# Windowed attention on one core: own keys and window keys in separate 128-column blocks

## Chip, cores and metric

One Trainium2 chip, one of its cores. The metric is the device time of one execution in microseconds; the median of the runs stands for a kernel. Profiled times count from the start of the span that the profiler records.

## What is computed

Two batches of 768 rows pass through an attention, a gated convolution block and a second one. Only the attention is touched by the change.

```
scores = scale * q @ k.T                       # 8 heads of 64
is_global = pos[None, :] < n_global            # 8
is_local  = (rel >= 0) & (rel < n_local)       # 96
dist = where(is_global & ~is_local, n_local, abs(rel))
scores = where(keep, scores - slopes * dist, -1e9)
a = softmax(scores)
x = a @ v                                      # attention
gate = sigmoid(causal conv(x)); y = (gate * (x @ w_val)) @ w_out
h = relu(y @ w_in); out = (h * sigmoid(conv(h))) @ w_out2
```

Query row r sees the 8 global keys and the last 96 rows up to itself.

## The kernel before

The 2 x 768 rows are 12 tiles of 128 queries, 6 a batch. For a tile the keys are 232: the previous tile's last 96 (PREV), the tile's own 128, and the 8 global ones (GLOB). For the first tile of a batch (tiles 0 and 6) they are 128. All matrix products are fp32, or split into a high and a low part.

The layout cuts the 232 keys of a tile in another place than the tiles do. kW holds previous 96, own 128, global 8 in this order. OLD = 104 of them are "old": the previous 96 and the tile's own first 8. The other NEW = 128 are the tile's own keys 8 to 127 and the global 8. Old keys are seen only by the tile's first 104 queries. So `turn` transposes the old part of each head as 104 x 104, and `pv` adds its product to 104 query columns only. v is stored to match: v_new (own rows 8 to 127, then the global 8) takes two loads, v_old (previous 96, own 8) two more. probT holds both parts of two heads side by side in 464 columns.

Each engine has its program written out by hand. One round t of the loop is, on TensorE, `qk(t + 1)` (scores of the next tile, 8 heads), `turn(t, j)` for four pairs of heads, `pv(t)`. VectorE takes the scores out of PSUM with bias and minimum (L951), copies turned pairs 1 and 3 (`copy_t1`, L958), takes x out (L974), and makes the inverse of the sums (total_eps L962, reciprocal, a small transpose). ScalarE does the exponentials (L701) and copies pairs 0 and 2 (L708). Three PSUM banks serve four pairs, so pair 3 waits for the copy of pair 0. GpSimd copies the window's keys from tile to tile (`key_window`, L384, L385), splits w2 (L397, L399), splits x for the next stage (L405, L407) and multiplies x by the inverse (`scale_x`, L391). SyncE issues all loads in one order; in a round it sends the inverse to memory, loads v, q and k of later tiles and loads the inverse back, spread out.

Ahead of the loop stands a product of two weights, w1t by win, on TensorE (L469, L454), fed by part loads on SyncE's and ScalarE's queues. SyncE waits for the third part of both (`w1_in[2]`) before it loads wval and the second half of win. VectorE makes the tables of biases in that time (L1057 to L1074), then low parts of weights (L931, L926). Behind the loop TensorE does dense products to the end.

Of the kernel before, what the change touches and what calls it, by code (L numbers as in the profile page):

```python
# [6 lines left out]
P = 128  # L7
C = H * D
# [11 lines left out]
KEYS = PREV + P + GLOB  # L20
OLD = PREV + GLOB
NEW = KEYS - OLD
BAND = PREV + P
# [20 lines left out]
def program(nc, A_q, A_k, A_v, A_n, A_wval, A_w1t, A_win, A_w2, A_cw1, A_cw2, A_out):  # L44
# [7 lines left out]
    with ctx:  # L52
# [62 lines left out]
        v_new = sb("v_new", [P, RING, C], where=am)  # L115
        v_old = sb("v_old", [P, RING, C], where=am)
# [5 lines left out]
        probT = sb("probT", [P, PAIRS, 512], where=am)  # L122
# [7 lines left out]
        rel, loc = probT[:, 0, 0:KEYS + GLOB], probT[:, 0, KEYS + GLOB:2 * (KEYS + GLOB)]  # L130
        notloc, lt = probT[:, 1, 0:KEYS + GLOB], probT[:, 1, KEYS + GLOB:2 * (KEYS + GLOB)]
        dist, dist_first = probT[:, 2, 0:KEYS], probT[:, 2, KEYS:KEYS + P]
        key, glob, dglob = (probT[:, 3, i * GLOB:(i + 1) * GLOB] for i in range(3))
# [134 lines left out]

        @block.sync
        def _(sp):  # L270
# [4 lines left out]
            sp.wait_ge(w1_in[2], 32)  # L275
# [958 lines left out]
```

## Time and profile before

| | us |
|---|---|
| median of 3 runs | 265.56 |
| lowest and highest | 265.42, 266.8 |
| the profiled execution's own time | 265.42 |
| its span | 263.6 |

| engine | busy us | share of the span |
|---|---|---|
| TensorE, matmul | 256.9 | 97% |
| TensorE, weight load | 203.7 | 77% |
| VectorE | 187.5 | 71% |
| ScalarE | 149.1 | 57% |
| GpSimd | 46.5 | 18% |

TensorE's granted clock is full over the whole span. An fp32 product shows as two records of weight load and two of matmul, a turn (transpose) as one of each. A matmul's duration holds its way through the array too, so for what one costs the others the starts are read, not the durations. Durations of GpSimd are rough.

### The profile page before, as it was taken

What the parts mean: (1) busy time and instruction counts of PE and PEld (TensorE: products, weight loads), DVE (VectorE), ACT (ScalarE), POOL (GpSimd) and SP (SyncE); (2) the same over time, 40 slices, a digit from 0 to 9 for tenths busy, and PEclk for the clock granted to TensorE, in tenths of its full rate; (3) what the DMA queues carried; (4) which work ended last, traced back from release to release, by engine and by line L of the source; (5) the groups of instructions that cost most, each with busy time, mean ns of one, the idle gap of its engine ahead of it and who ended that gap; (6) DMA issues with size and microseconds to landing.
All of it is one profiled execution on the core that took longest, in us unless ns stands there. A gap on an engine that the chain in (4) does not pass through costs nothing.

```text
span 263.6 us, 4429 instructions
## 1 busy us (share of the span) xinstructions
PE 256.9 (97%) x1526; PEld 203.7 (77%) x1526; DVE 187.5 (71%) x468; ACT 149.1 (57%) x346; POOL 46.5 (18%) x71
## 2 busy tenths in 40 slices
PE   8999999999999899999999999999999999999995
PEld 7544468889678788888888888888888888888883
DVE  0388389998999969989833979987319989991000
ACT  1061578999989755263634328965447559752100
POOL 1002157793568512000000000000000000000000
PEclk9999999999999999999999999999999999999999
DMA  6799957779785111000000000000000004004021
GB/s 203 258 357 275 308 169 223 222 211 258 224 260 149 46 55 31 2 1 2 0 0 0 0 2 0 1 0 2 0 0 0 2 0 159 0 0 162 0 107 53
DMA packets 24635, 24.67 MB, mean 94 GB/s; under 512 B 3732, under 2 KB 16532, under 8 KB 24484
## 3 DMA queue, kind: packets, MB, share of 16 engines
q1 hardware_dynamic: 23460, 23.37, 29.2%
q10 hardware_dynamic: 1152, 1.01, 1.1%
q8 instruction: 13, 0.21, 0.3%
q14 instruction: 10, 0.08, 0.1%
HBM read 21.03 MB, written 3.34 MB: 92 GB/s over the span
## 4 chain that ended last, share of the span: by engine, by line
PE 88%; DVE 8%; issue 2%; ACT 1%; ACTq 0%
PE ps L561 21%; PE ps L563 21%; PE ps L562 21%; PE ps L454 9%; PE ps L501 4%; DVE prob L951 4%; PE ps L528 4%; PE ps L515 2%; PE ps L532 2%; PE ps L516 2%; PE ps L469 1%; PE ps L465 1%; DVE total_eps L962 1%; DVE probT L958 1%; DVE xT L974 1%
## 5 line engine op out<-in xcount | busy, mean ns | idle before, releaser
L701 ACT ACTIVATE prob<-prob,low 128x232 f32<-128x232 f32 (+1 forms) x96 | 44.3, 466 | 6.9 <-DVE low L951 6.7
L979 DVE SCALAR_TENSOR_TENSOR g<-xT,cw,g 128x512 f32<-128x512 f32 x48 | 34.9, 793 | 1.6 <-ACT g L736 1.6
L807 ACT ACTIVATE h<-ps 128x512 f32<-128x512 f32 x24 | 14.0, 596 | 31.2 <-PE ps L563 31.1
L951 DVE CUSTOM_DVE_ANT_0 prob<-ps,bias 128x232 f32<-128x232 f32 x80 | 28.4, 383 | 1.4 <-PE ps L501 1.3
L561 PE MATMUL ps<-gh,Wh 128*128 128x512 f32 x64 | 24.9, 389 | 0.0
L562 PE MATMUL ps<-gl,Wh 128*128 128x512 f32 x64 | 24.9, 389 | 0.0
L563 PE MATMUL ps<-gh,Wl 128*128 128x512 f32 x64 | 24.9, 389 | 0.0
L561 PE MATMUL ps<-hghA,w2h 128*128 128x512 f32 x64 | 24.9, 389 | 0.0
L562 PE MATMUL ps<-hglA,w2h 128*128 128x512 f32 x64 | 24.9, 389 | 0.0
L563 PE MATMUL ps<-hghA,w2l 128*128 128x512 f32 x64 | 24.9, 389 | 0.0
L454 PE MATMUL ps<-win,w1t 128*128 128x512 f32 x56 | 24.5, 594 | 0.0
L1141 DVE SCALAR_TENSOR_TENSOR hgA<-h,cw,hgA 128x512 f32<-128x512 f32 x32 | 21.8, 745 | 3.6 <-ACT hgA L819 3.6
L501 PE MATMUL ps<-kW,q_rows 64*128 64x232 f32 (+1 forms) x192 | 20.7, 355 | 0.0
L516 PE MATMUL ps<-ident,prob 128*128 128x128 f32 x96 | 20.3, 275 | 0.4 <-ACT probT L708 0.3
L454 PEld LDWEIGHTS ps<-win,w1t 128*128 128x128 f32 x56 | 10.6, 190 | 12.6 <-issue 12.4
L528 PE MATMUL ps<-probT,v_new 128*64 128x128 f32 x192 | 19.3, 282 | 1.0 <-DVE probT L958 0.9
L561 PE MATMUL ps<-xh,wvh 128*128 128x512 f32 x48 | 19.0, 395 | 0.3 <-issue 0.3
L501 PEld LDWEIGHTS ps<-kW,q_rows 64*128 64x128 f32 x192 | 16.6, 186 | 3.0 <-issue 1.1
L562 PE MATMUL ps<-xl,wvh 128*128 128x512 f32 x48 | 18.7, 390 | 0.0
L563 PE MATMUL ps<-xh,wvl 128*128 128x512 f32 x48 | 18.7, 390 | 0.0
L515 PE MATMUL ps<-ident,prob 104*104 104x104 f32 x80 | 17.8, 260 | 0.9 <-ACT probT L708 0.9
L701 ACT ACTIVATION_READ_ACCUMULATOR prob<-prob,low 128x1 f32 x96 | 18.3, 191 | 0.0
(105 smaller groups left out, 545.6 us busy)
## 6 DMA issues: line engine op xcount, KB each, us to landing
q_rows<-in_q SPq DMA_DIRECT2D x12, 256.0 KB, 4.3
kW<-in_k SPq DMA_DIRECT2D x12, 256.0 KB, 5.0
v_new<-in_v SPq DMA_DIRECT2D x12, 240.0 KB
invT<-inv_turned SPq DMA_DIRECT2D x20, 128.0 KB, 3.3
out<-xT SPq DMA_DIRECT2D x5, 512.0 KB, 2.8
w<-in_w SPq DMA_DIRECT2D x8, 256.0 KB, 9.7
v_old<-in_v SPq DMA_DIRECT2D x10, 192.0 KB
prob<-in_wval SPq DMA_DIRECT2D x1, 1024.0 KB, 4.8
```

The costliest lines, as they stand in the source:

```text
L454: return pe.matmul(WB(i), w1t[:, m, k * P:(k + 1) * P], win[:, m, half * 512:(half + 1) * 512], start=(m == 0), stop=(m == CT - 1))
L501: last = pe.matmul(SC(f, i % 2)[:, i // 2, OLD if first_of_batch(t) else 0:KEYS], q_rows[rows, slot, pair, :], keys, start=True, stop=True)
L515: pe.transpose(PT(t, j)[0:OLD, at:at + OLD], head[0:OLD, 0:OLD], ident[0:OLD, 0:OLD])
L516: last = pe.transpose(PT(t, j)[:, at + OLD:at + KEYS], head[:, OLD:KEYS], ident[:, :])
L528: last = pe.matmul(PO[rows, j, :], v_new[:, slot, cols], probT[:, j, e * KEYS + OLD:(e + 1) * KEYS], start=True, stop=first_of_batch(t))
L561: pe.matmul(out, w_hi, x_hi, start=first, stop=False)
L562: pe.matmul(out, w_hi, x_lo, start=False, stop=False)
L563: return pe.matmul(out, w_lo, x_hi, start=False, stop=final)
L701: act.activation(part, part, ACT.Exp, scale=-1.0, bias=low[:, t % 2, i:i + 1], accum_out=total[:, t % 2, i:i + 1]).then_inc(exp_done, 1)
L951: dve.tensor_tensor_reduce(prob[:, t % 2, i, cols], SC(f, e)[:, i % HH // 2, cols], table, -SCALE, 3.0e38, ALU.add, ALU.min, low[:, t % 2, ...
L979: dve.scalar_tensor_tensor(out=pieces(g[:, m, :], c), in0=x_cols(m, c, tap - PAD1), scalar=cw1[:, m, tap:tap + 1], in1=pieces(g[:, m, :], ...
L1141: dve.scalar_tensor_tensor(out=raw, in0=h_cols(m, c, tap - 1), scalar=cw2[:, m, tap:tap + 1], in1=raw, op0=ALU.mult, op1=ALU.add).then_inc ...
```

## The change

The keys of a tile are cut where the tiles are cut. The window (WIN = 104) is now the global 8 and the previous 96, the rest are the tile's own 128 keys in their order. kW holds window and own part in that order. v is held as v_own (128 rows, one load) and v_win (96 and 8 rows, two loads); the first tile of a batch has v_own only. The turned parts lie in blocks of 128 columns: `turn` transposes the 104 window keys for all 128 queries, and `pv` multiplies window and own part for all 128 queries, the window first. The copies out of PSUM take 512 columns where they took 464. The tables of biases are built over other slices, with one operation and one iota fewer. SyncE's wait for `w1_in[2]` ahead of wval is gone.

```diff
 GLOB, PREV = 8, 96
-KEYS = PREV + P + GLOB
-OLD = PREV + GLOB
-NEW = KEYS - OLD
-BAND = PREV + P
+WIN = GLOB + PREV
+KEYS = WIN + P
...
-        probT = sb("probT", [P, PAIRS, 512], where=am)
+        probT = sb("probT", [P, HALVES, HH, 2, P], where=am)
...
         def turned(t, j):
-            both = PT(t, j)[:, 0:2 * KEYS]
-            return both.rearrange("p (i k) -> p i k", i=2)[:, :, OLD:KEYS] if first_of_batch(t) else both
+            rows = PT(t, j).rearrange("p (i c q) -> p i c q", i=2, c=2)
+            return rows[:, :, 1, :] if first_of_batch(t) else rows.rearrange("p i c q -> p (i c q)")
...
-            sp.wait_ge(w1_in[2], 32)
             sp.dma_start(wval, A_wval).then_inc(wv_in, 16)
...
-                sp.dma_start(v_new[0:P - GLOB, slot, :], A_v[GLOB:P, t, :]).then_inc(v_in[slot], 16)
-                sp.dma_start(v_new[P - GLOB:P, slot, :], A_v[0:GLOB, t // TPB * TPB, :]).then_inc(v_in[slot], 16)
+                sp.dma_start(v_own[:, slot, :], A_v[:, t, :]).then_inc(v_in[slot], 16)
                 if not first_of_batch(t):
-                    sp.dma_start(v_old[0:PREV, slot, :], A_v[P - PREV:P, t - 1, :]).then_inc(v_in[slot], 16)
-                    sp.dma_start(v_old[PREV:OLD, slot, :], A_v[0:GLOB, t, :]).then_inc(v_in[slot], 16)
+                    sp.dma_start(v_win[GLOB:WIN, slot, :], A_v[P - PREV:P, t - 1, :]).then_inc(v_in[slot], 16)
+                    sp.dma_start(v_win[0:GLOB, slot, :], A_v[0:GLOB, t // TPB * TPB, :]).then_inc(v_in[slot], 16)
...
                 for i in range(2):
-                    head, at = prob[:, t % 2, 2 * j + i, :], i * KEYS
-                    if not first_of_batch(t):
-                        pe.transpose(PT(t, j)[0:OLD, at:at + OLD], head[0:OLD, 0:OLD], ident[0:OLD, 0:OLD])
-                    last = pe.transpose(PT(t, j)[:, at + OLD:at + KEYS], head[:, OLD:KEYS], ident[:, :])
+                    for c in key_parts(t):
+                        keys = slice(WIN, KEYS) if c else slice(0, WIN)
+                        last = pe.transpose(PT(t, j)[0:keys.stop - keys.start, (2 * i + c) * P:(2 * i + c + 1) * P],
+                                            prob[:, t % 2, 2 * j + i, keys], ident[:, :])
...
-                    heads = [(e, slice((2 * j + e) * D, (2 * j + e + 1) * D), slice(e * D, (e + 1) * D)) for e in range(2)]
-                    for e, cols, rows in heads:
-                        last = pe.matmul(PO[rows, j, :], v_new[:, slot, cols], probT[:, j, e * KEYS + OLD:(e + 1) * KEYS],
-                                         start=True, stop=first_of_batch(t))
-                    if not first_of_batch(t):
-                        for e, cols, rows in heads:
-                            last = pe.matmul(PO[rows, j, 0:OLD], v_old[0:OLD, slot, cols], probT[0:OLD, j, e * KEYS:e * KEYS + OLD],
-                                             start=False, stop=True)
+                    for c in key_parts(t):
+                        v, keys = (v_win, v_own)[c], (WIN, P)[c]
+                        for e in range(2):
+                            cols = slice((2 * j + e) * D, (2 * j + e + 1) * D)
+                            last = pe.matmul(PO[e * D:(e + 1) * D, j, :], v[0:keys, slot, cols], probT[0:keys, j // 2, j % 2 * 2 + e, c, :],
+                                             start=(c == key_parts(t)[0]), stop=(c == 1))
...
-                link(dve.scalar_tensor_tensor(out=dist[:, 0:BAND], in0=notloc[:, 0:BAND], scalar=MASKED,
-                                              in1=loc[:, 0:BAND], op0=ALU.mult, op1=ALU.add))
-                link(dve.tensor_copy(dist[:, BAND:KEYS], dglob))
-                link(dve.tensor_copy(dist_first[:, 0:BAND - OLD], dist[:, OLD:BAND]))
-                link(dve.tensor_tensor(dist_first[:, BAND - OLD:NEW], notloc[:, KEYS:KEYS + GLOB], dglob, ALU.mult))
-                link(dve.tensor_tensor(dist_first[:, BAND - OLD:NEW], dist_first[:, BAND - OLD:NEW], loc[:, KEYS:KEYS + GLOB], ALU.add))
+                link(dve.tensor_tensor(dist_first, notloc[:, own], dglob, ALU.mult))
+                link(dve.tensor_tensor(dist_first, dist_first, loc[:, own], ALU.add))
+                link(dve.tensor_copy(dist[:, 0:GLOB], dglob[:, 0:GLOB]))
+                link(dve.scalar_tensor_tensor(out=dist[:, window_keys], in0=notloc[:, window_keys], scalar=MASKED,
+                                              in1=loc[:, window_keys], op0=ALU.mult, op1=ALU.add))
```

TensorE, tile 1, the last turns and the first two pairs of `pv`, before. A row names the line, the output and the inputs, and the output's rows by columns; "x2" is two heads.

```order
L515 MATMUL ps<-ident,prob 104x104
L516 MATMUL ps<-ident,prob 128x128
L528 MATMUL ps<-probT,v_new 64x128 x2
L532 MATMUL ps<-probT,v_old 64x104 x2
L528 MATMUL ps<-probT,v_new 64x128 x2
```

The same place in the changed kernel:

```order
L517 MATMUL ps<-ident,prob 104x128
L517 MATMUL ps<-ident,prob 128x128
L532 MATMUL ps<-probT,v_win 64x128 x2
L532 MATMUL ps<-probT,v_own 64x128 x2
L532 MATMUL ps<-probT,v_win 64x128 x2
```

The count is the same; the window part comes first in `pv`, and its rows go from 104 to 128 columns.

SyncE, one round's loads with the inverse's way out and back (L303, L311), before:

```order
L303 DMA inv_turned<-inv_rows 4x32x32
L294 DMA v_new<-in_v 120x512
L295 DMA v_new<-in_v 8x512
L297 DMA v_old<-in_v 96x512
L298 DMA v_old<-in_v 8x512
L283 DMA q_rows<-in_q 128x512
L288 DMA kW<-in_k 128x4x128
L311 DMA invT<-inv_turned 64x4x128 x2
```

The same round in the changed kernel:

```order
L307 DMA inv_turned<-inv_rows 4x32x32
L299 DMA v_own<-in_v 128x512
L301 DMA v_win<-in_v 96x512
L302 DMA v_win<-in_v 8x512
L288 DMA q_rows<-in_q 128x512
L293 DMA kW<-in_k 128x4x128
L315 DMA invT<-inv_turned 64x4x128 x2
```

One load stands fewer ahead of q, k and the inverse.

## Rows read from the trace of the kernel before

**Rows 1.** The page's chain that ended last: shares of the span by engine.

```profile
PE 88%; DVE 8%; issue 2%; ACT 1%; ACTq 0%
```

**Rows 2.** Busy time by stretch: length, then each engine (x instructions), clock, DMA share, GB/s.

```profile
43.89:49.27 5.38, 5.38 (x67) 4.68 (x66) 4.89 (x22) 4.88 (x19) 3.96 (x6) 1.00 0.82 235
...
64.75:70.13 5.38, 4.89 (x46) 3.56 (x48) 5.01 (x23) 4.98 (x20) 2.23 (x4) 1.00 0.82 231
70.13:75.45 5.32, 5.21 (x64) 4.26 (x60) 5.29 (x22) 5.10 (x18) 3.44 (x5) 1.00 0.82 239
...
107.00:250.00 143.00, 143.00 (x633) 118.44 (x632) 103.81 (x146) 76.77 (x106) 0.00 (x0) 1.00 0.04 15
```

**Rows 3.** Timeline of the weight loads in round 7: start, us, what, [idle before].

```profile
73.97 0.20 PEld L528 LDWEIGHTS ps<-probT,v_new 128*64 128x64 f32 x4 [0.31 <-DVE probT L958]
```

**Rows 4.** Timeline of TensorE in round 2, three turns in a row.

```profile
45.84 0.25 PE L515 MATMUL ps<-ident,prob 104*104 104x104 f32 x1
45.93 0.27 PE L516 MATMUL ps<-ident,prob 128*128 128x128 f32 x1
46.04 0.25 PE L515 MATMUL ps<-ident,prob 104*104 104x104 f32 x1
```

**Rows 5.** The chain at 92 us: start, us, what.

```profile
92.02 0.18 PE ps L532 x4
92.20 0.22 PE ps L528 x4
```

**Rows 6.** Groups by line and shape: the copies out of PSUM on VectorE.

```profile
L958 DVE COPY probT<-ps 128x464 f32<-128x464 f32 x20 | 12.8, 639 | 2.5 <-PE ps L516 2.4
...
L958 DVE COPY probT<-ps 128x256 f32<-128x256 f32 x4 | 1.7, 419 | 0.0
```

**Rows 7.** Timeline of VectorE in rounds 6 to 10: total_eps and one conv step.

```profile
66.42 0.85 DVE L962 TENSOR_SCALAR total_eps<-total 128x8 f32<-128x8 f32 x1
...
71.35 1.09 DVE L962 TENSOR_SCALAR total_eps<-total 128x8 f32<-128x8 f32 x1
...
77.13 0.17 DVE L962 TENSOR_SCALAR total_eps<-total 128x8 f32<-128x8 f32 x1
...
82.80 0.85 DVE L962 TENSOR_SCALAR total_eps<-total 128x8 f32<-128x8 f32 x1
...
86.86 1.69 DVE L979 SCALAR_TENSOR_TENSOR g<-xT,cw,g 128x512 f32<-128x512 f32 x1
```

**Rows 8.** Timeline of GpSimd in the same rounds.

```profile
65.97 1.28 POOL L391 TENSOR_TENSOR xT<-xT,invT 128x512 f32<-128x512 f32 x1 [0.56 <-DMA invT<-inv_turned]
...
71.13 1.28 POOL L407 TENSOR_TENSOR xl<-xT,xh 128x512 fp32r<-128x512 f32 x1
...
77.23 1.28 POOL L407 TENSOR_TENSOR xl<-xT,xh 128x512 fp32r<-128x512 f32 x1
...
86.73 1.27 POOL L391 TENSOR_TENSOR xT<-xT,invT 128x512 f32<-128x512 f32 x1
```

**Rows 9.** Timeline of SyncE's queue in round 6, one of four v loads.

```profile
69.07 0.31 SPq L295 DMA_DIRECT2D v_new<-in_v  x1
```

**Rows 10.** The start: timeline rows, one DMA issue, and one group by shape.

```profile
7.93 17.33 PE L454 MATMUL ps<-win,w1t 128*128 128x512 f32 x40
...
9.40 0.33 SPq L276 DMA_DIRECT2D prob<-in_wval  x1
...
21.78 3.07 DVE L926 TENSOR_TENSOR Wl<-ps,Wh 128x512 fp32r<-128x512 f32 x5
...
25.19 0.97 PEld L501 LDWEIGHTS ps<-kW,q_rows 64*128 64x128 f32 x16 [0.76 <-DVE Wl L926]
...
33.34 1.48 PEld L501 LDWEIGHTS ps<-kW,q_rows 64*128 64x128 f32 x16 [0.76 <-issue]
...
prob<-in_wval SPq DMA_DIRECT2D x1, 1024.0 KB, 4.8
...
L1057 DVE TENSOR_SCALAR probT<-probT,nval 128x240 f32<-128x240 f32 x1 | 0.3, 345 | 2.6 <-POOL probT L414 2.6
```

More of the change, by code:

```diff
@@ L114, in program @@
         q_rows = sb("q_rows", [P, RING, PAIRS, P], where=am)
-        v_new = sb("v_new", [P, RING, C], where=am)
-        v_old = sb("v_old", [P, RING, C], where=am)
+        v_own = sb("v_own", [P, RING, C], where=am)
+        v_win = sb("v_win", [P, RING, C], where=am)
         bias = sb("bias", [P, H, KEYS], where=am)
@@ L129, in program @@
         wval = prob[:, :, :, :].rearrange("p s i k -> p (s i k)")[:, 2 * H * KEYS - CT * C:2 * H * KEYS].rearrange("p (t c) -> p t c", t=CT)
[L130 to L133, printed above, removed]
+        rel = probT[:, 0, 0:2, :, :].rearrange("p a b c -> p (a b c)")[:, 0:KEYS]
+        loc = probT[:, 0, 0:2, :, :].rearrange("p a b c -> p (a b c)")[:, KEYS:2 * KEYS]
+        notloc = probT[:, 0, 2:4, :, :].rearrange("p a b c -> p (a b c)")[:, 0:KEYS]
+        key = probT[:, 0, 2:4, :, :].rearrange("p a b c -> p (a b c)")[:, KEYS:2 * KEYS][:, 0:P]
+        glob = probT[:, 1, 0:2, :, :].rearrange("p a b c -> p (a b c)")[:, 0:P]
+        dglob = probT[:, 1, 0:2, :, :].rearrange("p a b c -> p (a b c)")[:, P:2 * P]
+        lt = probT[:, 1, 0:2, :, :].rearrange("p a b c -> p (a b c)")[:, KEYS:2 * KEYS]
+        dist = probT[:, 1, 2:4, :, :].rearrange("p a b c -> p (a b c)")[:, 0:KEYS]
+        dist_first = probT[:, 1, 2:4, :, :].rearrange("p a b c -> p (a b c)")[:, KEYS:KEYS + P]
         attention_memory.close()
@@ L255, in first_of_batch, with key_parts @@
             return t % TPB == 0
+        def key_parts(t):
+            return (1,) if first_of_batch(t) else (0, 1)
         def v_landed(t):
-            return 16 * sum(2 if first_of_batch(u) else 4 for u in range(t % RING, t + 1, RING))
+            return 16 * sum(1 if first_of_batch(u) else 3 for u in range(t % RING, t + 1, RING))
         def turned(t, j):
-            both = PT(t, j)[:, 0:2 * KEYS]
-            return both.rearrange("p (i k) -> p i k", i=2)[:, :, OLD:KEYS] if first_of_batch(t) else both
+            rows = PT(t, j).rearrange("p (i c q) -> p i c q", i=2, c=2)
+            return rows[:, :, 1, :] if first_of_batch(t) else rows.rearrange("p i c q -> p (i c q)")
         def turned_to(t, j):
-            both = probT[:, j, 0:2 * KEYS]
-            return both.rearrange("p (i k) -> p i k", i=2)[:, :, OLD:KEYS] if first_of_batch(t) else both
+            part = probT[:, j // 2, j % 2 * 2:j % 2 * 2 + 2, :, :]
+            return part[:, :, 1, :] if first_of_batch(t) else part.rearrange("p i c q -> p (i c q)")
         @block.sync
@@ L499, in qk @@
                         pair, rows = 2 * f + i // 2, slice(i % 2 * D, i % 2 * D + D)
-                        keys = kW[rows, slot, pair, OLD if first_of_batch(t) else 0:KEYS]
-                        last = pe.matmul(SC(f, i % 2)[:, i // 2, OLD if first_of_batch(t) else 0:KEYS], q_rows[rows, slot, pair, :], keys,
+                        keys = kW[rows, slot, pair, P if first_of_batch(t) else P - WIN:2 * P]
+                        last = pe.matmul(SC(f, i % 2)[:, i // 2, WIN if first_of_batch(t) else 0:KEYS], q_rows[rows, slot, pair, :], keys,
                                          start=True, stop=True)
@@ L1055, in _ @@
             with dve.If(banded(dve)):
-                dve.wait_ge(iotas, 3)
+                dve.wait_ge(iotas, 2)
+                own, window_keys = slice(WIN, KEYS), slice(GLOB, KEYS)
                 link(dve.tensor_scalar(lt, rel, n_local, None, ALU.is_lt))
```

20 lines of the change are left out of this document (9 added, 11 removed).

## Prediction

> **What bounds the kernel now.** I read the chain of waits first, to see which engine carries the end [rows 1]. TensorE has 88% of it, VectorE 8%, so I asked next in which stretches VectorE stands in it. I call "round t" what TensorE does in one step of the attention loop: the scores of tile t+1, the turns (transposes) of tile t, its product with v. The busy time by stretch [rows 2] gives round 2 (43.89 to 49.27 us): TensorE 5.38 of 5.38 us, VectorE 4.89. Rounds 1 to 5 are like it. In rounds 6 (64.75) and 7 (70.13) TensorE has gaps, VectorE is busy 5.01 and 5.29 us and ScalarE 4.98 and 5.10: there the chain runs over VectorE. A wait of 0.31 us of TensorE for VectorE's copy in round 7 shows it [rows 3]. Behind the loop TensorE is busy 143.00 of 143.00 us [rows 2], so whatever the attention loop gains or loses by then reaches the end in full.
>
> **TensorE's columns.** For the ten tiles that have a window (all but 0 and 6) the key part of 104 is turned with 128 moving columns instead of 104, and the v part gets 128 query columns instead of 104. The timeline of round 2 shows three starts [rows 4]: the 104-column turn at 45.84, the 128-column one at 45.93, the next 104-column one at 46.04. So a turn of 104 columns holds the engine 0.09 us and one of 128 columns 0.11 us. Eight heads by 0.02 is 0.16 us a tile. In the chain [rows 5], four records of v_old (two heads side by side, 104 columns) take 0.18 us, four of v_new (128 columns) 0.22. Four pairs by 0.04 is 0.16 us. The last turn pair of a round waits about 0.1 us for ScalarE's copy of the first, since it reuses its PSUM bank; the added columns fill about 0.04 of that. A windowed tile costs TensorE 0.16 + 0.16 - 0.04 = 0.28 us. That the v_own product now follows v_win, and that accumulation starts with the window, changes no count and no weight; I cost it at nothing, with bounds of 0.02 us a pair either way, the size of the gaps that the rows can't resolve.
>
> Another reading of these gaps would be that weight loads set them: then the turns would stay as they are, and the sum would be 0.12 us less in each of rounds 1 to 5, 8 and 11, some 0.85 us. Against it: the short gap of 0.09 us is the one in which the 128 weight columns of the next turn are loaded, and the long one of 0.11 that in which 104 are. The Trainium skill, "TensorE: Matmul & The Clock Gate", section "LDWEIGHTS (loading the stationary operand)", has a load take its columns over 1.2 GHz, whatever the rows: an estimate of 107 ns for 128 columns and 87 for 104. By it the turns would cost nothing more. The trace has the long and the short gap the other way round, so I don't follow it here.
>
> **The copies out of PSUM.** They grow from 464 to 512 columns. VectorE takes 639 ns at 464 columns and 419 at 256 [rows 6]: 1.06 ns a column, so 48 more are 0.05 us each, two a tile. ScalarE's copies grow by the same columns, and I take the same 0.05, two a tile. For tiles 0 and 6 they stay at 2 x 128. In round 2 VectorE has 5.38 - 4.89 = 0.49 us of room, and the round gets 0.28 longer, so the copies hide.
>
> **The path, round by round.** Rounds 1 to 5 are TensorE's: 5 x 0.28 = 1.40. Round 0 and round 6 turn first tiles: nothing. In round 7 TensorE waits for VectorE's copies: two copies (0.10) and the last product (0.04), 0.14. Over rounds 8 to 10 the chain goes from TensorE to VectorE in round 9 and stays there until the last scores of tile 11 free the banks for the next stage: two copies in each of rounds 8 to 10, less what waited for TensorE anyway, 3 x 0.10 and up to 0.10 of turns ahead of a copy: 0.40. Tile 11 is turned between dense products, on TensorE alone: 0.28. Sum 1.40 + 0.14 + 0.40 + 0.28 = 2.22 us.
>
> **The port that VectorE and GpSimd share.** VectorE's total_eps works on 8 columns and should take some 0.17 us, as in round 8 (77.13). It took 0.85 in round 6 and 1.09 in round 7, and the conv step (usually 0.79) took 1.69 in round 10 [rows 7]. In rounds 6 and 7 it ends at 67.27 and 72.44, right where GpSimd's tensor_tensor ends (65.97 + 1.28 = 67.25; 71.13 + 1.28 = 72.41); in round 10 the conv step starts 0.13 us after GpSimd's multiply at 86.73 [rows 8]. These waits are 0.68 + 0.92 + 0.90 us, with one of 0.68 in round 9 (0.85 at 82.80) like them, and all four stand in the chain. What sets GpSimd's phase is in the diff: each of its operations there follows a k tile or an inverse that SyncE sends, after the v loads of the same step. One v load fewer takes 0.31 us off SyncE's queue [rows 9]. And two rounds of TensorE that are 0.28 longer lie between the moment GpSimd's inverse for round 6 is sent and VectorE's total_eps there. So GpSimd comes 0.31 + 0.56 = 0.87 us earlier against VectorE; its multiply started 0.45 us before total_eps and ran 0.83 into it, so the wait of round 6 should be gone. Not all of that reaches the end: the exponentials on ScalarE, busy 4.98 and 5.10 us in rounds 6 and 7, keep the next total_eps from following, and in round 7 it still meets a GpSimd operation. I take 0.64 us for both rounds (of 0.68 in round 6, with round 7's collision kept at what ScalarE leaves), between nothing and 1.6 (both waits).
>
> The Trainium skill has this as a rule, in "SBUF — State Buffer", section "Who interferes with whom": VectorE and GpSimd share one port pair as an exclusive lock, and whichever comes first keeps it for its whole instruction. By that rule, the trace agrees: 0.85 and 1.09 us for an operation of 0.17, each ending with the GpSimd one.
>
> **SyncE and the start.** Without its wait, wval is issued at about 3.1 us instead of 9.40 [rows 10]. It stands behind all w1t parts in SyncE's own queue, so only the last halves of win on ScalarE's queue can be slowed. TensorE needs the third part at 11.4 and the fourth at 14.8 us (7.93 + 8 and 16 records of 0.43); the wait removed ended at 9.40, so the third had 2 us of room. wval and q, k, v of the first tiles come up to 3 us earlier, but no engine in the chain waited for them: TensorE runs through its 40 records from 7.93 at 0.43 each. The tables of biases lose one link, but five operations go from 8 to 128 columns. One of 240 takes 345 ns [rows 10], one of 8 took 170 [rows 7], so 120 more cost about 0.09 us, or 0.45 for the five, less the link's 0.2: VectorE gets there about 0.3 us later. TensorE's first scores start after a gap of 0.76 us "for VectorE"; the same gap of 0.76 us stands before the second tile's scores with no wait, so it is the engine's own. The fourth Wl, for which the first scores wait, ended at about 24.3 (21.78 and four steps of 0.6), some 0.8 us before their start at 25.19, and that hides it. Start: 0. Upper bound: wval took 4.8 us to land; if it held up the third part by all of that, 9.4 + 4.8 - 11.4 = 2.8 us.
>
> **Sum.** 265.42 us is the profiled execution's own time (its span of 263.6 and 1.8 around it); 265.42 + 2.22 - 0.64 = 267.0 us. That execution lies 0.14 below the median of 265.56.
>
> **The rivals.**
> - The port waits stay or form anew. For it: in round 8 total_eps started at 77.13, just 0.1 us before GpSimd's tensor_tensor at 77.23 [rows 7, 8]; with GpSimd 0.31 us or more earlier it comes just behind it and waits up to 1.2 us, of which TensorE has little to hide. Against: what is formed there is won in round 6. 265.42 + 2.22 = 267.6 with the waits as they are, 268.5 with a new one of 0.9. Chance 0.27.
> - More of them go. GpSimd's multiply in round 10 also comes after a chain of GpSimd work that begins with a k tile; started 0.9 us earlier, as in round 6, it is half over before the conv step. Price up to -0.9 more: 266.1. Chance 0.20.
> - The other side, not slower at all: TensorE's added columns stay, but all four waits (3.18 us) go; it decides once more than 2.2 us of them are gone. 265.42 + 2.22 - 3.18 = 264.5. ScalarE's load in rounds 6 and 7 speaks against. Chance 0.05 for 264.0 to 265.4.
> - The columns don't cost what the gaps say (weight loads bind the turns): 267.0 - 0.85 = 266.1. Chance 0.06.
> - The start: wval delays the win parts and TensorE by up to 2.8 us: 268 to 269.8. It decides from 2 us of delay of the third part. Chance 0.04.
>
> **How the numbers follow.** The forecast, 266.6 to 267.3, has 0.38. A measurement of this kernel tells about 0.5% from no change, here 264.2 to 266.9. The forecast's own case falls about half on either side of 266.9: slower gets 0.20 + 0.27 + 0.04 = 0.51, the same 0.18 + 0.20 + 0.06 + 0.03 = 0.47, faster 0.02. The range runs from 265.7 (the relief of 266.1 with the column terms a little smaller) to 268.5 (a new wait).
>
> **What would show it.** Turns of 104 by 128 spaced 0.11 us and v pairs of 0.22 + 0.22; rounds 1 to 5 at 5.66 us; VectorE copies of 0.69 us; first scores still at 25.2 and the second at 33.3 us; total_eps near 0.2 us in round 6. Wrong would be: rounds 1 to 5 still at 5.4 us (columns free), a first score later than 25.5 (start), or waits of total_eps in rounds 6 to 9 that sum to more than the 2.28 us of before.

## The result, and the profile after

The changed kernel takes 267.86 us (median of 12 runs, 267.32 to 270.44) against 265.45 (12 runs, 264.09 to 266.8) for the kernel before: a ratio of 1.011, with a 95% interval of 1.008 to 1.0142. The ratios here and below come from the runs of both kernels and not from the two medians, which stand at 1.009 here; a few high runs count in them. The forecast was 267.0 in 265.7 to 268.5, most likely slower. The profiled execution of after has a span of 268.7 us and a time of 270.46, the top of its runs. So the comparison of the two profiles shows more than the medians do, and I come back to where the surplus lies.

The page of after: the head, the busy times, and the chain that ended last (compare [rows 1]).

```profile
span 268.7 us, 4415 instructions
...
PE 260.6 (97%) x1526; PEld 206.1 (77%) x1526; DVE 188.6 (70%) x467; ACT 150.1 (56%) x346; POOL 46.6 (17%) x70
...
PE 80%; DVE 10%; DMA 3%; ACT 2%; issue 2%; DVEq 1%; ACTq 0%
```

DMA was not in the chain of before. It is now, with 3%. The busy time by stretch of after (length, then TensorE, weight loads, VectorE, ScalarE, GpSimd, clock, DMA share, GB/s), from the start to the first scores, then rounds 2, 3, 6 and 7, and all behind the loop; compare [rows 2]:

```profile
0.00:28.48 28.48, 25.46 (x70) 14.09 (x70) 13.50 (x41) 6.96 (x11) 3.04 (x14) 1.00 0.93 285
...
47.38:53.40 6.02, 5.91 (x66) 4.85 (x64) 5.57 (x21) 5.02 (x19) 3.86 (x6) 1.00 0.68 181
53.40:59.05 5.65, 5.65 (x66) 4.90 (x64) 5.29 (x24) 5.01 (x19) 5.41 (x8) 1.00 0.87 259
...
69.68:73.93 4.25, 4.12 (x43) 3.14 (x41) 3.81 (x19) 3.77 (x16) 1.26 (x1) 1.00 0.66 209
73.93:80.04 6.11, 5.74 (x66) 4.89 (x64) 5.90 (x26) 6.11 (x23) 3.72 (x5) 1.00 0.89 248
...
98.04:268.70 170.66, 167.47 (x768) 138.38 (x768) 114.61 (x163) 85.83 (x123) 3.21 (x5) 1.00 0.06 22
```

A clean round is 5.65 us, TensorE busy in all of it (5.38 before). Round 2 is 6.02 with gaps in TensorE. The end of round 6 comes early (4.25 us), and round 7 is then 6.11, with ScalarE busy in every one of the 6.11. The clock is the full one throughout.

I cut each kernel's trace into five parts by the first weight load of the scores. "Wait" is what total_eps took beyond its 0.17 us, summed over rounds 1 to 10; waits of other instructions, the conv step above all, are not in it. All in us, one profiled execution each. Cut so, rounds 6 and 7 of before are 4.93 and 5.78 (in [rows 2] the cut between them is half a us later; the sum is the same). The kernels from the third row on are those of the next section.

| kernel | first scores | rounds 1–5 | 6+7 | 8–10 | behind the loop | wait |
|---|---|---|---|---|---|---|
| before | 25.19 | 26.24 | 10.71 | 17.86 | 170.36 | 2.93 |
| after | 28.48 | 27.95 | 10.36 | 18.00 | 170.66 | 2.84 |
| a_wait (after, wait of wval back) | 25.27 | 28.23 | 10.36 | 18.68 | 170.62 | 4.45 |
| after_again | 26.44 | 27.70 | 10.64 | 18.43 | 170.64 | 4.24 |
| b_nowait (before, no wait) | 26.12 | 26.24 | 10.19 | 18.41 | 170.38 | 2.74 |
| b_noeps (before, no total_eps) | 25.46 | 26.24 | 10.12 | 16.18 | 170.40 | none |
| aw_noeps (a_wait, no total_eps) | 25.91 | 27.58 | 10.35 | 17.19 | 170.68 | none |

After against before, in the two profiles: start +3.29, rounds 1 to 5 +1.71, rounds 6 and 7 −0.35, rounds 8 to 10 +0.14, the rest +0.30; together 5.09 of the 5.1 us between the spans. The loop and what follows it gives 1.8, close to the 1.58 forecast; the start gives 3.3 where I forecast 0.

**The start.** Timeline of the start of after (start, us, what, [idle before]), with the chain's first piece, and three DMA issues of its page (KB each, median us from issue to landing):

```profile
3.08 0.43 SPq L281 DMA_DIRECT2D prob<-in_wval  x1
...
11.48 0.17 DVE L935 CAST nf<-nw 128x4 f32<-128x4 int32 x1 [10.47 <-DMA nw<-in_n]
...
13.94 14.00 PE L456 MATMUL ps<-win,w1t 128*128 128x512 f32 x32 [1.42 <-DMA win<-in_win]
...
28.48 0.97 PEld L503 LDWEIGHTS ps<-kW,q_rows 64*128 64x128 f32 x16 [1.37 <-DVE Wl L926]
```

```profile
2.15 9.30 DMA nw<-in_n
```

```profile
prob<-in_wval SPq DMA_DIRECT2D x1, 1024.0 KB, 12.0
...
win<-in_win ACTq DMA_DIRECT2D x3, 256.0 KB, 11.3
...
nw<-in_n ACTq DMA_DIRECT2D x1, 2.0 KB, 9.3
```

wval goes out at 3.08 us (9.40 before) and needs 12.0 us to land (4.8 before, [rows 10]). The transfers beside it are stretched: win on ScalarE's queue from 6.7 to 11.3 us, the 2 KB load of nw from 5.6 to 9.3. TensorE starts its first full product late (8.92 against 7.93; three runs with the wait, further down, start it at 8.79 to 8.96, so this part need not come from wval) and then stands 1.42 us for win, which it never did before. The product so ends at 27.94 instead of 25.26, 2.7 us late. The other 0.6 us is VectorE's: nw came 3.7 us late, the tables behind it too, and the low parts Wl, begun at 21.78 in before, begin at 25.96 here, so TensorE's gap before the first scores is 1.37 us for Wl where it had been 0.76. That is the path by which DMA, with nw, comes into the chain.

**The loop.** Timeline of after (compare [rows 7, 8]): GpSimd and VectorE in round 2, total_eps of round 6, GpSimd and VectorE in round 8:

```profile
49.01 1.28 POOL L395 TENSOR_TENSOR xT<-xT,invT 128x512 f32<-128x512 f32 x1
...
49.13 1.19 DVE L962 TENSOR_SCALAR total_eps<-total 128x8 f32<-128x8 f32 x1
...
71.43 0.17 DVE L962 TENSOR_SCALAR total_eps<-total 128x8 f32<-128x8 f32 x1
...
81.34 1.27 POOL L411 TENSOR_TENSOR xl<-xT,xh 128x512 fp32r<-128x512 f32 x1
...
81.79 0.85 DVE L962 TENSOR_SCALAR total_eps<-total 128x8 f32<-128x8 f32 x1
```

GpSimd's multiply starts 0.12 us ahead of total_eps and ends at 50.29; total_eps ends at 50.32. That is the rival "form anew", in a round where I had not looked for it. It also came where I had named it: in round 8 total_eps is 0.85 us where it had been 0.17, and ends at 82.64, GpSimd's operation at 82.61. In round 6, where 0.85 us had been, it is 0.17, as forecast.

### The profile page after: what moved, and what is told of

Same layout as the page of the kernel before. It is cut to its first block, busy times and chain, and to the rows that moved or that the text cites. A ratio compares the mean times of both kernels' runs of the same rounds, so it can differ in the third digit from the quotient of the medians.

```text
span 268.7 us, 4415 instructions
## 1 busy us (share of the span) xinstructions
PE 260.6 (97%) x1526; PEld 206.1 (77%) x1526; DVE 188.6 (70%) x467; ACT 150.1 (56%) x346; POOL 46.6 (17%) x70
## 3 DMA queue, kind: packets, MB, share of 16 engines
q10 hardware_dynamic: 1152, 1.01, 1.2%
## 4 chain that ended last, share of the span: by engine, by line
PE 80%; DVE 10%; DMA 3%; ACT 2%; issue 2%; DVEq 1%; ACTq 0%
PE ps L561 20%; PE ps L563 20%; PE ps L562 20%; PE ps L532 7%; PE ps L517 5%; PE ps L503 5%; DMA nw<-in_n 3%; PE ps L456 3%; DVE prob L951 2%; ACT prob L701 1%; DVE Wl L926 1%; DVE bias L1075 1%; DVE wvl L931 1%; DVE total_eps L962 1%; DVE probT L958 1%
## 5 line engine op out<-in xcount | busy, mean ns | idle before, releaser
L517 PE MATMUL ps<-ident,prob 128*128 128x128 f32 (+1 forms) x176 | 23.1, 277 | 1.4 <-ACT probT L708 1.3
L517 PEld LDWEIGHTS ps<-ident,prob 128*128 128x128 f32 (+1 forms) x176 | 18.7, 136 | 6.3 <-issue 2.7
L532 PE MATMUL ps<-probT,v_own 128*64 128x128 f32 x192 | 18.3, 274 | 0.4 <-DVE probT L958 0.4
```

What stands on the lines that cost most here:

```text
L517: last = pe.transpose(PT(t, j)[0:keys.stop - keys.start, (2 * i + c) * P:(2 * i + c + 1) * P], prob[:, t % 2, 2 * j + i, keys], ident[:, :])
L532: last = pe.matmul(PO[e * D:(e + 1) * D, j, :], v[0:keys, slot, cols], probT[0:keys, j // 2, j % 2 * 2 + e, c, :], start=(c == key_parts(t ...
```

## The experiments

The bracketed time is the kernel before on the same chips. Times are medians of all runs of a kernel; ratios have their 95% interval.

### Is the surplus the columns or the start?

**a_wait**: the changed kernel with SyncE's wait back.

```diff
+            sp.wait_ge(w1_in[2], 32)
             sp.dma_start(wval, A_wval).then_inc(wv_in, 16)
```

> The changed kernel with SyncE's wait for w1_in[2] ahead of wval put back. Theory 'start' (wval, let loose at 3.1 us, takes the DMA engines from the loads ahead of it, nw and the win parts, by an amount that differs from run to run): first scores back at 25.2 us, the runs lie close together, median 267.2 to 267.5 and no run above 268.3; in the profile the loop alone is about 1.5 to 2.2 us longer than before. Theory 'loop' (the late start of the one profile is chance, all of the 2.4 us is columns, copies and port waits): median 267.9 like the changed kernel's, and runs up to 270 as there.

267.96 us (267.52 to 268.27, 6 runs) [265.28]; ratio 1.0096 (1.0067 to 1.0126). First scores at 25.27, as in before:

```profile
8.01 17.33 PE L457 MATMUL ps<-win,w1t 128*128 128x512 f32 x40
...
25.27 0.97 PEld L504 LDWEIGHTS ps<-kW,q_rows 64*128 64x128 f32 x16 [0.76 <-DVE Wl L927]
```

So the slowdown of 1% is there without the late start, and with the start of before. But the port waits were more, in rounds 2, 3 and 4; its busy time by stretch for those three, then VectorE and GpSimd in round 4:

```profile
44.16:50.01 5.85, 5.85 (x67) 4.86 (x65) 5.40 (x21) 5.01 (x19) 4.37 (x7) 1.00 0.69 189
50.01:55.80 5.79, 5.79 (x66) 4.84 (x64) 5.57 (x23) 5.06 (x19) 4.98 (x7) 1.00 0.75 213
55.80:61.77 5.97, 5.91 (x66) 4.85 (x65) 5.74 (x23) 5.07 (x19) 5.81 (x7) 1.00 0.63 185
```

```profile
57.33 1.28 POOL L404 TENSOR_TENSOR w2l<-w,w2h 128x512 fp32r<-128x512 f32 x1
...
57.55 1.08 DVE L963 TENSOR_SCALAR total_eps<-total 128x8 f32<-128x8 f32 x1
```

Again one ends with the other (58.61 and 58.63). Three rounds that would be 5.65 are 5.85, 5.79 and 5.97: 0.66 us from three waits of 0.84, 0.80 and 0.91.

**b_nowait**: the kernel before without the wait, nothing else.

```diff
-            sp.wait_ge(w1_in[2], 32)
             sp.dma_start(wval, A_wval).then_inc(wv_in, 16)
```

> The kernel before with only the wait taken away. Theory 'start': first scores between 25.2 and 28.5 us; the times spread upwards, median 265.5 to 266.3 and some runs at 267 to 268.7. Theory 'loop': 265.45 within 0.3, spread as before, first scores at 25.2.

266.03 us (264.23 to 267.16, 12 runs) [265.28]; ratio 1.0013 (0.9983 to 1.0043). Rounds 1 to 5 are those of before. The start is not:

```profile
8.86 17.33 PE L453 MATMUL ps<-win,w1t 128*128 128x512 f32 x40
...
26.12 0.97 PEld L500 LDWEIGHTS ps<-kW,q_rows 64*128 64x128 f32 x16 [0.76 <-DVE Wl L925]
```

TensorE's product starts 0.9 us later, but without a gap: this time win was there. The late start is not shown to come from the wait's removal either: in b_turn128, b_pv128 and b_copy512, which keep the wait, the product starts at 8.96, 8.85 and 8.79. In time the wait's removal cannot be told from nothing.

**after_again**: the changed kernel once more, as it is.

> The changed kernel once more, for a second profile and more times beside the three above on the same chip. Theory 'start': another profile has its first scores anywhere from 25.2 to 28.5, and its own time goes with that, 267.4 plus the shift. Theory 'loop': the first scores vary without the time following.

268.28 us (266.89 to 268.88, 6 runs) [265.28]; ratio 1.0101 (1.0068 to 1.0134). First scores at 26.44, so most of the 3.3 us at the start of the first profile belongs to that one execution. Nor is its round 6 that of the first profile: total_eps takes 0.58 us there, and rounds 6 and 7 are 10.64 us, hardly less than before. Of the 12 runs of the first measurement four lay at 269.06 to 270.44, eight at 267.32 to 268.03; a late win of 1 to 2 us in some executions would look like that, but only the one at the top has a trace.

**a_nwfirst**: the changed kernel with nw's load at the head of ScalarE's queue.

```diff
+            act.dma_start(nw[:, :], A_n.partition_broadcast(P)).then_inc(n_in, 16)
             act.dma_start(w1t[:, 0, 0:P], A_w1t[:, 0, 0:P]).then_inc(start_in[0], 16)
...
-                if m == 1:
-                    act.dma_start(nw[:, :], A_n.partition_broadcast(P)).then_inc(n_in, 16)
```

> The changed kernel (no wait), with the 2 KB load of nw issued first on ScalarE's queue, ahead of the weight parts. Theory 'start by nw' (the late landing of nw holds back the tables of VectorE, and these the first scores): nw lands before 5 us, first scores at 25.5 to 26.6, where only the idle time of TensorE for a win part is left; median 267.2 to 267.6. Theory 'start by win' (the late win part is what counts): first scores as in the changed kernel's profile, 28.5, and no gain.

269.06 us (267.03 to 269.63, 4 runs) [265.28]; ratio 1.0116 (1.0069 to 1.0163). nw is there 8 us earlier and the first scores are still late:

```profile
3.54 0.17 DVE L934 CAST nf<-nw 128x4 f32<-128x4 int32 x1 [2.53 <-DMA nw<-in_n]
...
10.67 17.33 PE L456 MATMUL ps<-win,w1t 128*128 128x512 f32 x40
...
27.93 0.97 PEld L503 LDWEIGHTS ps<-kW,q_rows 64*128 64x128 f32 x16 [0.76 <-issue]
```

With the tables early, the scores wait for the big product alone, which could run only from 10.67 here and had no gap. In this one profile w1t's first part, now behind nw, lands 3.7 us after its issue (2.5 in after), and TensorE waits 0.49 us for it. So an early nw alone did not bring the first scores back; of the 0.6 us that the late tables cost in after's profile this run says nothing.

### What is a column worth, part by part?

**b_turn128**: the kernel before, whose turns of the old part take 128 moving columns.

```diff
-                        pe.transpose(PT(t, j)[0:OLD, at:at + OLD], head[0:OLD, 0:OLD], ident[0:OLD, 0:OLD])
+                        pe.transpose(PT(t, j)[0:OLD, at:at + P], head[:, 0:OLD], ident[:, :])
```

> The kernel before, with the 104-key turns given 128 moving columns (the 24 more are overwritten by the second turn). Theory 'moving columns': turns spaced 0.11 instead of 0.09 us, rounds 1 to 5 at 5.50 us (0.16 less the 0.04 that was waited), time +0.9 (266.3 to 266.4). Theory 'weight loads': spacing and time as before.

265.94 us (264.5 to 267.35, 12 runs) [265.12]; ratio 1.0025 (1.0003 to 1.0047).

**b_pv128**: the kernel before, whose v_old products take 128 columns (24 of them come from the neighbouring block, so this part of the output is another).

```diff
-                            last = pe.matmul(PO[rows, j, 0:OLD], v_old[0:OLD, slot, cols], probT[0:OLD, j, e * KEYS:e * KEYS + OLD],
+                            last = pe.matmul(PO[rows, j, :], v_old[0:OLD, slot, cols], probT[0:OLD, j, e * KEYS:e * KEYS + P],
```

> The kernel before, with v_old's product over all 128 queries (the last 24 take wrong factors, so that part of the output isn't the reference's). Theory 'moving columns': v pairs of 0.44 instead of 0.40 us, rounds 1 to 5 at 5.54, time +1.1 to +1.3 (266.6 to 266.8). Rival: two heads side by side hide the 24 columns, 265.5.

266.68 us (265.73 to 268.4, 12 runs) [265.12]; ratio 1.0062 (1.0039 to 1.0085).

**b_copy512**: the kernel before, whose copies out of PSUM take 512 columns.

```diff
-            return both.rearrange("p (i k) -> p i k", i=2)[:, :, OLD:KEYS] if first_of_batch(t) else both
+            return both.rearrange("p (i k) -> p i k", i=2)[:, :, OLD:KEYS] if first_of_batch(t) else PT(t, j)
```

> The kernel before, with the copies out of PSUM over 512 columns instead of 464 (the 48 more are not used). Theory 'hidden in rounds 1 to 5': those stay at 5.38 us, rounds 7 to 10 grow by 0.05 to 0.10 each, time +0.3 (265.5 to 265.9). Rival 'copies on the path everywhere': +1.0, 266.5.

265.78 us (265.36 to 267.83, 12 runs) [265.12]; ratio 1.0025 (1.0001 to 1.0048).

The busy time by stretch of one round without port waits each (round 3 of b_turn128 and b_pv128, round 1 of b_copy512), then round 2 of b_copy512 and what happened in it:

```profile
44.92:50.37 5.45, 5.45 (x66) 4.78 (x64) 4.96 (x22) 4.87 (x19) 3.27 (x5) 1.00 0.80 226
```

```profile
44.90:50.44 5.54, 5.54 (x66) 4.80 (x64) 4.89 (x22) 4.87 (x19) 4.21 (x6) 1.00 0.80 224
```

```profile
39.30:44.72 5.42, 5.42 (x66) 4.68 (x64) 5.39 (x26) 5.03 (x19) 2.71 (x5) 1.00 0.69 200
44.72:50.73 6.01, 5.77 (x67) 4.72 (x65) 5.57 (x22) 5.21 (x19) 4.09 (x7) 1.00 0.69 189
```

```profile
46.37 1.28 POOL L391 TENSOR_TENSOR xT<-xT,invT 128x512 f32<-128x512 f32 x1
...
46.47 1.22 DVE L962 TENSOR_SCALAR total_eps<-total 128x8 f32<-128x8 f32 x1
```

Against 5.38, the turns cost a round 0.07, the v products 0.16, the copies 0.04: together 0.27, the 5.65 of after. Round 1 of b_copy512 has no port wait, and its copies are yet not hidden. Where the 0.04 comes from shows at the last pair of turns, which waits for ScalarE's copy; TensorE in round 1, first before, then b_copy512:

```profile
41.36 0.27 PE L516 MATMUL ps<-ident,prob 128*128 128x128 f32 x1
41.56 0.27 PE L515 MATMUL ps<-ident,prob 104*104 104x104 f32 x1
```

```profile
42.22 0.27 PE L516 MATMUL ps<-ident,prob 128*128 128x128 f32 x1
42.46 0.27 PE L515 MATMUL ps<-ident,prob 104*104 104x104 f32 x1
```

The step is 0.20 us in before and 0.24 in b_copy512, where 0.11 is what it takes without a wait. By their ratios the three cost +0.66, +1.64 and +0.66 us, in sum 2.96; a_wait, which has all three, was at +2.55 with an interval of 1.8 to 3.3. b_copy512 also has waits of 1.05 and 1.07 us in rounds 2 and 4 that before doesn't have, and a round of 6.01 from it. Between the two kernels total_eps of round 2 and GpSimd's multiply moved by 0.26 us against one another: it starts 0.16 us ahead of the multiply in before (45.57 and 45.73), 0.10 behind it here. That is more than the 0.04 a round, and b_pv128, whose rounds are 0.16 longer, keeps it ahead. All four profiles with total_eps and copies of 464 columns have it ahead (by 0.10 to 0.19), six of the seven with 512 have it behind (by 0.09 to 0.32), after_again alone ahead by 0.04. So this wait goes with the longer copies; by what path they move GpSimd against VectorE isn't shown.

### What do the port waits cost, and does the change cost more through them?

**b_noeps**: the kernel before, the reciprocal taken from total itself; the 1e-9 added against a zero sum is left out.

```diff
-                dve.tensor_scalar(total_eps[:, :], total[:, t % 2, :], 1e-9, None, ALU.add).then_inc(total_done, 1)
-                dve.wait_ge(total_done, t + 1)
-                dve.reciprocal(inv[:, 0:H], total_eps[:, :]).then_inc(reciprocal_done, 1)
+                dve.reciprocal(inv[:, 0:H], total[:, t % 2, :]).then_inc(reciprocal_done, 1)
```

> The kernel before without total_eps: the reciprocal is taken of the sum itself (the sums are at least 1, where adding 1e-9 changes nothing in fp32). Theory 'port': the waits of 0.44, 0.68, 0.92 and 0.68 us in rounds 0, 6, 7, 9 go, and of these 1.0 to 2.0 us reach the end: 263.5 to 264.5. Rival 'ScalarE holds those rounds': under 0.5 us reaches the end, 265.0 or more.

263.55 us (262.63 to 264.76, 12 runs) [265.12]; ratio 0.9936 (0.9914 to 0.9959). This is the fastest of all the kernels here, 1.6 us below before. Its rounds 0, 3, 6, 7 and 10:

```profile
33.62:38.06 4.44, 4.14 (x42) 3.13 (x41) 3.67 (x19) 3.10 (x12) 3.71 (x4) 1.00 0.19 67
...
43.44:48.82 5.38, 5.38 (x66) 4.68 (x64) 4.72 (x21) 4.87 (x19) 3.73 (x6) 1.00 0.81 235
...
64.30:68.44 4.14, 4.01 (x43) 3.16 (x41) 3.73 (x18) 3.81 (x15) 1.92 (x3) 1.00 0.92 239
68.44:74.42 5.98, 5.45 (x66) 4.68 (x64) 5.14 (x25) 5.98 (x24) 3.93 (x6) 1.00 0.91 251
...
85.19:90.60 5.41, 5.41 (x66) 4.68 (x64) 5.41 (x23) 4.90 (x19) 4.36 (x4) 1.00 0.19 55
```

Round by round against before: round 0 −0.65, rounds 6 and 7 −0.59 together, rounds 8 to 10 −1.68. In round 7 ScalarE is busy all 5.98 us: with no port wait left, it is what holds rounds 6 and 7 at 10.12. Of the 1.68 us, 1.23 lie in round 10 (6.64 to 5.41), where before has no wait of total_eps but the conv step's 1.69 us of [rows 7]; in b_noeps no conv step of these rounds takes more than 0.93. So the edit also moved that collision out of the way, and the gain is not that of total_eps's own waits alone. The gain in time, 1.6 us, is less than the 2.9 that the loop lost in the profile (59.90 to 56.98 us from the second scores on); the profiled execution of b_noeps, 262.76, is 0.8 below its median.

The rule of the Trainium skill that the prediction leaned on ("SBUF — State Buffer", "Who interferes with whom": VectorE and GpSimd share a port pair as an exclusive lock) was told there without its limits: the section has a VectorE instruction with at most one input in SBUF contend only in a mode that uses both ports, which a tensor_scalar such as total_eps can enter, and has one with two inputs in SBUF, such as the conv step, contend with a GpSimd instruction that reads SBUF. With these limits the trace agrees: the reciprocal of the same 8 columns, with one input, is not held up (0.19 to 0.21 us in all rounds, also at 82.67 in after, while a GpSimd multiply runs from 82.57 to 83.85), and with total_eps taken away the waits don't move to it.

**aw_noeps** and **a_noeps**: the same edit in the changed kernel, with SyncE's wait and without it.

> The changed kernel with SyncE's wait put back and without total_eps (the reciprocal of the sums themselves). Theory 'columns and copies': beside the kernel before without total_eps (263.55 us) only the work terms are left, rounds 1 to 4 at 5.65 us against 5.38 and rounds 8 to 10 at 5.65 too; about 2.4 us more, 265.9 to 266.2. Theory 'port': if the difference of the two kernels was made by the waits of total_eps, it shrinks to under 1 us, 264.5.

> The changed kernel as it is (no wait of SyncE), without total_eps. Theory 'start counts': first scores 1 to 3 us later than with the wait in one run or another, so the median lies 0.5 to 1.5 us above the one with the wait and the spread is wider. Theory 'start is chance either way': the same within 0.3 us.

aw_noeps 265.89 us (265.22 to 266.57, 12 runs) [265.69]; ratio 1.0009 (0.9978 to 1.004). a_noeps 266.19 us (265.32 up, one outlier at 374.75, 12 runs) [265.69]; ratio 1.0024 (0.9996 to 1.0051). Every round of 1 to 4 is now 5.65 in both. Round 3 and round 9 of aw_noeps, then GpSimd and VectorE at the start of round 9:

```profile
44.20:49.85 5.65, 5.65 (x68) 4.89 (x66) 4.83 (x21) 4.96 (x20) 4.36 (x7) 1.00 0.81 235
...
82.08:87.98 5.90, 5.75 (x67) 4.89 (x65) 5.90 (x23) 4.85 (x19) 5.49 (x5) 1.00 0.19 54
```

```profile
81.54 1.27 POOL L412 TENSOR_TENSOR xl<-xT,xh 128x512 fp32r<-128x512 f32 x1
...
81.84 1.52 DVE L978 SCALAR_TENSOR_TENSOR g<-xT,cw,g 128x512 f32<-128x512 f32 x1
```

So one port wait is left in aw_noeps: the conv step, 0.75 us otherwise, takes 1.52 behind GpSimd's operation, and round 9 is 5.90 where its neighbours are 5.65 and 5.64. (In a_noeps it is 1.82 and the round 6.19.)

Without total_eps the change costs 1.0009 / 0.9936, some 0.73% or 1.9 us, the two ratios with 0.3% and 0.2% either way; the loops of the two profiles differ by 59.56 − 56.98 = 2.58 us (rounds 1 to 5 1.34, 6 and 7 0.23, 8 to 10 1.01, of which 0.25 is the conv step's wait). With total_eps it costs, by the ratios of a_wait, after_again and after, 2.5 to 2.9 us. So the added work is most of the loss; that the port waits add 0.6 to 1.0 us to it lies within the intervals. The wait of wval is 0.3 us between the two, again not resolved.

**aw_2loads**: a_wait with v_own in two loads, so that SyncE has as many v loads as before.

```diff
-                sp.dma_start(v_own[:, slot, :], A_v[:, t, :]).then_inc(v_in[slot], 16)
+                sp.dma_start(v_own[GLOB:P, slot, :], A_v[GLOB:P, t, :]).then_inc(v_in[slot], 16)
+                sp.dma_start(v_own[0:GLOB, slot, :], A_v[0:GLOB, t, :]).then_inc(v_in[slot], 16)
```

> The changed kernel with SyncE's wait put back and v_own loaded in two parts (120 and 8 rows), so that each round has four v loads again. Theory 'phase by the queue': GpSimd's work comes about 0.3 us later against VectorE, total_eps meets other operations in rounds 2 to 9 and the sum of its waits differs by over 0.5 us from the 3.9 us with three loads; the time moves by 0.3 to 1.0 us, either way. Rival: one load more changes neither, 267.8 to 268.1.

267.59 us (266.5 to 268.87, 12 runs) [265.69]; ratio 1.0081 (1.0051 to 1.011). The waits of rounds 1 to 10 sum to 3.35 us against a_wait's 4.45, with round 4 free of one and round 2 still at 0.81; round 6 is 4.25 us as in after. The time is not to be told from a_wait's, so whether a load moves the waits by more than one execution differs from the next stays open.

**aw_104**: a_wait with the own part first and the window part for 104 queries only, in turn and product (the window's share of the last 24 queries is left out of the output).

```diff
+                        q = P if c else WIN
-                        last = pe.transpose(PT(t, j)[0:keys.stop - keys.start, (2 * i + c) * P:(2 * i + c + 1) * P],
-                                            prob[:, t % 2, 2 * j + i, keys], ident[:, :])
+                        last = pe.transpose(PT(t, j)[0:keys.stop - keys.start, (2 * i + c) * P:(2 * i + c) * P + q],
+                                            prob[0:q, t % 2, 2 * j + i, keys], ident[0:q, 0:q])
...
-                    for c in key_parts(t):
+                    for c in key_parts(t)[::-1]:
```

> The changed kernel with SyncE's wait put back, whose window part is turned and multiplied for the first 104 queries only, own part first (the global keys of the last 24 queries are left out, so that part isn't the reference's). Layout, v loads and 512-column copies stay as changed. Theory 'columns': rounds 1 to 4 at 5.42 us, as in the kernel before with 512-column copies, time 265.6 to 266.0. Rival 'layout' (new addresses, one v load fewer, phase of GpSimd): stays at 267 or more.

266.9 us (264.62 to 267.68, 12 runs) [265.69]; ratio 1.0044 (1.0014 to 1.0075). The clean rounds are 5.42 and 5.43 us, as b_copy512's; so of a clean round's 0.27 the columns on TensorE are 0.23, which is b_turn128's 0.07 and b_pv128's 0.16; the order of the two products costs nothing. Two weight loads of scores mark where its round 2 begins and ends:

```profile
43.99 1.48 PEld L504 LDWEIGHTS ps<-kW,q_rows 64*128 64x128 f32 x16
...
49.99 1.48 PEld L504 LDWEIGHTS ps<-kW,q_rows 64*128 64x128 f32 x16
```

6.00 us, with a port wait of 1.04. The time lies between what the two theories expected (up to 266.0, and 267 or more), and this is one place where it went.

## Why the prediction was right, and where it was not

The number (267.0 for 267.86) and the side were right; several of its parts were not, and the misses partly cancel, so some of the hit is luck. Step by step:

- **TensorE's columns, 0.28 a tile: right in sum, not in parts.** Clean rounds went from 5.38 to 5.65 and what is behind the loop (with tile 11's turns) by 0.30. The v products are 0.16 as worked out. Turns cost 0.07 on the path where I had 0.12: more of the added columns than the 0.04 I allowed fill the wait for ScalarE's copy that stood there before. The rival "weight loads set the gap" fell with b_turn128: round 5.45, time 1.0025 (1.0003 to 1.0047). So did the use of the Trainium skill beside it ("TensorE: Matmul & The Clock Gate", "LDWEIGHTS (loading the stationary operand)"): the section has a load's time go by its columns alone. Taken for the gap between turns, the trace doesn't agree: b_turn128 leaves the 104 weight columns of the old part as they are, and all its turns are 0.11 us apart, where [rows 4] had 0.09 and 0.11. The chain of after, round 3, turns then products (compare [rows 4, 5]); 16 turns in 1.97 us are 0.12 each, 32 products in 1.91 us 0.06 each:

```profile
55.24 1.97 PE ps L517 x16
57.21 1.91 PE ps L532 x32
```

- **The copies hide: wrong, by 0.04 a round.** Their size was right (forecast 0.69; the groups by shape of after, where the second is ScalarE's, 550 ns before):

```profile
L958 DVE COPY probT<-ps 128x512 f32<-128x512 f32 x20 | 13.8, 688 | 2.7 <-PE ps L517 2.5
...
L708 ACT ACTIVATE probT<-ps 128x512 f32<-128x512 f32 x20 | 11.8, 591 | 4.5 <-PE ps L517 4.5
```

  I compared VectorE's busy time with the round and found room. The copy that counts is ScalarE's of the first pair, 0.04 longer (forecast 0.05), which TensorE's last pair waits for, since it takes the same bank: 0.24 us in b_copy512 where it was 0.20. I had used that wait in the line above and not asked what the longer copy does to it. The two errors (0.05 too much, 0.04 too little) cancel.

- **Rounds 8 to 10, 0.40: too small, and hidden by the waits.** They were to be 0.40 longer: 0.14 in after, 0.82 in a_wait, 0.57 in after_again, with other port waits in each. Between b_noeps and aw_noeps they differ by 1.01 us (16.18 to 17.19): 0.26, 0.52 and 0.23 a round. In the first and the last TensorE is busy all the time and takes its added columns in full; the middle one is round 9 with the conv step's wait, 0.25 of it. Without port waits the term is so about 0.76, where I had worked out 0.40 on a path over VectorE. Round 7's 0.14 was nearer: rounds 6 and 7 differ by 0.23 between the same two. The conv step's wait of round 10, which the forecast kept, is 1.69 us at 86.86 in before, 1.53 at 85.95 in after and 1.76 at 83.46 in a_wait, both in round 9, and gone in after_again (0.90): the collision is not tied to one round.

- **Relief in rounds 6 and 7, −0.64: it came in one profile, and the reason given isn't shown.** In after total_eps of round 6 is 0.17 us, and rounds 6 and 7 are 0.35 shorter, where −0.64 + 0.14 made −0.50. In after_again, the same kernel, total_eps takes 0.58 and the rounds are 0.07 shorter. And b_nowait, with neither a load fewer nor a column more, has the same round 6 (4.24 us, against 4.93), so has b_pv128 (4.25), which keeps the old loads, and so has aw_2loads (4.25). The step "0.31 us off SyncE's queue plus 0.56 us of TensorE, so GpSimd comes 0.87 us earlier" isn't shown by any of them. More likely, though not shown, the wait in before's profile belongs to that one execution: in the two profiles of the changed kernel total_eps of round 2 starts 0.12 us behind GpSimd's multiply and 0.04 ahead of it. What caps the gain was right: ScalarE, busy 6.11 of 6.11 in round 7.

- **No new wait in rounds 1 to 5: wrong.** I had searched the port's rows from round 6 on, where TensorE had gaps, and named round 8. There it came (0.68 in after, 1.13 in a_wait, 1.07 in after_again), but not there alone. Before itself has 0.38 and 0.21 in rounds 3 and 4, at no cost to the round. In after, rounds 2 and 3 have waits of 1.02 and 0.21; in a_wait rounds 2 to 4 have 0.84, 0.80 and 0.91; after_again has 0.72 in round 4. A wait of 0.7 to 1 costs a round of the changed kernel 0.1 to 0.4 us, and one of b_copy512 0.6. Rounds 1 to 5 so gave 1.71 in after and 1.99 in a_wait, for 1.40; without port waits they give 1.34. The rival "form anew" gave 267.6 to 268.5, and 267.86 lies in it: by its mechanism this rival, which I gave 0.27, holds as much of the case as the forecast. My mark against the forecast, waits of over 2.28 us in rounds 6 to 9, was not reached in after (1.61) and a_wait (1.90), but in after_again (3.52).

- **The start costs nothing: wrong in the trace, not resolved in the time.** By my own mark (a first score later than 25.5) it failed: 28.48 in after, and 26.12, 26.29 and 26.44 in b_nowait, a_noeps and after_again. With the wait it was 24.99 to 26.22 in nine kernels, so my mark was drawn too close, and of the five starts without it only 28.48 and a_nwfirst's 27.93 stand clear of that spread. The failed step was "2 us of room for the third part": in after TensorE stood 1.42 us after eight records, right where that part is due. I counted wval's 4.8 us of landing against the last parts of win only, but without the wait it lands in 9.6 to 12.0, and the three 256 KB parts of win beside it in 7.5 to 11.3 (median of the three), for 6.3 to 6.8 in the nine kernels with the wait. nw's 9.3 us stands in after alone; in b_nowait, a_noeps and after_again it is 5.8 to 6.4, with the wait 5.2 to 5.9. The start of TensorE's whole product is no sure sign either: 8.86 to 9.18 without the wait (10.67 with nw first), 7.73 to 8.96 with it. The rival's upper bound of 2.8 us was too low for after's profile (3.3). In time the wait's removal is +0.13% (−0.17 to +0.43) on before, and on after 267.86 against 267.96 with it.

What stays open is why the first scores come late in only some executions, and what the port waits cost in the median of after: each profile has its own set of them.

## What to carry to other kernels

On an engine that is busy in every us of a round, the cost of added columns can be read from the gaps between starts (the v products' 0.16 us came out as worked out), less what a wait beside them takes up, which is easily misjudged (the turns' 0.07 for 0.12); the phases between engines can't, and a shift of 0.26 us turned a harmless neighbour into a wait of 1 us here. So look for collisions over all rounds, not only those with gaps, and if a small operation waits for a port again and again, try to remove the operation rather than retime its neighbours: here that was worth 1.6 us, more than half of what the change cost, though another instruction can still collide. Room for a copy is to be sought at the one instruction that waits for it, not in the engine's busy share; and a large load issued early can stretch those in flight beside it (win's parts here), even where, as in this case, the time doesn't resolve what that costs.

## What the runs showed of the hardware beyond that

Between VectorE and GpSimd it is not the size of the operation that counts: an addition on 8 columns took 0.17 us alone and up to 1.30 (a_wait, round 8) when it came behind a GpSimd operation of 1.28, while the reciprocal of the same 8 columns right behind it stayed at 0.19 to 0.21. The conv step, on 512 columns, was held up too, 1.47 to 1.82 us for 0.75. And 256 KB loads on one queue took 7.5 to 11.3 us to land beside a 1 MB load of another queue, 6.3 to 6.8 without it.
